# Splitting the second MLP weight matrix on GpSimd beside the attention, by way of a DRAM scratch

## The reference

```python
# attention: 2 batches x 8 heads, 768 rows, head size 64
mask = q_bucket[:, :, :, None] == k_bucket[:, :, None, :]   # buckets: signs of q @ proj and k @ proj, 6 bits
scores = np.where(mask, scale * (q @ k^T), -1e9)
attn = exp(scores - max) / (sum + 1e-9);  x = attn @ v      # as 1536 tokens x 512
# MLP: w_in 512 x 2048, w_out 2048 x 512
h = x @ w_in
g = (a0 + a1*h + a2*h^2 + a3*h^3) / (1 + |b0|*|h| + |b1|*h^2 + 1e-6)
x2 = g @ w_out
# experts: each token goes to the one of 8 experts with the highest logit
out = gate * sigmoid(x2 @ w_output_gate) * (relu(x2 @ w1[e]) @ w2[e])
```

## Time and profile before

| | us |
|---|---|
| median of three runs | 840.91 |
| lowest, highest | 838.65, 841.00 |
| the profiled execution | 839.78 |
| its span, first to last instruction | 837.9 |
| TensorE busy | 784.2 (94%) |
| VectorE busy | 661.4 (79%) |
| ScalarE busy | 586.8 (70%) |
| GpSimd busy | 346.9 (41%) |
| mean granted TensorE clock | 0.979 of full speed |

### The profile page before, as it was taken

The page is one execution under the profiler, slowest core; times in us unless marked ns, Lnnn a source line. Parts: engine busy times, 40 slices in busy tenths (PEclk is TensorE's granted clock), DMA queues, the critical chain, the costliest instruction groups (busy, mean ns, idle before and its releaser), DMA issues.

```text
span 837.9 us, 16486 instructions
## 1 busy us (share of the span) xinstructions
PE 784.2 (94%) x5008; PEld 676.1 (81%) x5008; DVE 661.4 (79%) x1097; ACT 586.8 (70%) x1042; POOL 346.9 (41%) x320
## 2 busy tenths in 40 slices
PE   3599999999998799999999999999799999999995
PEld 2488888888887688899999999978588888888884
DVE  2477777777776699887878778767799999999982
ACT  1366766667676588886776777752599888888873
POOL 4055564664654222221221222220266656566452
PEclk9799999999999999999999999998899999999998
DMA  3566787786954421010010000023783112515940
GB/s 95 108 143 141 160 180 142 170 181 141 188 120 113 114 87 40 1 38 1 0 38 0 0 13 25 0 100 140 257 295 125 50 38 85 194 53 190 363 142 0
DMA packets 75652, 89.49 MB, mean 107 GB/s; under 512 B 34468, under 2 KB 51620, under 8 KB 75621
## 3 DMA queue, kind: packets, MB, share of 16 engines
q1 hardware_dynamic: 72580, 80.97, 36.1%
q0 software_dynamic: 3040, 8.13, 3.0%
HBM read 108.82 MB, written 8.18 MB: 140 GB/s over the span
## 4 chain that ended last, share of the span: by engine, by line
PE 87%; DVE 4%; issue 2%; ACT 2%; DMA 2%; SPq 1%; POOL 1%; DVEq 0%; POOLq 0%; ACTq 0%
PE ps_s L585 15%; PE ps_t L753 12%; PE ps_s L730 12%; PE ps_t L603 10%; PE ps_o L515 8%; PE ps_t L501 7%; PE ps_o L603 5%; PE ps_s L486 4%; PE ps_s L488 4%; PE ps_s L739 2%; PE ps_p L471 2%; PE ps_p L464 1%; DVE mask_st L991 1%; PE ps_o L717 1%; PE ps_p L644 1%
## 5 line engine op out<-in xcount | busy, mean ns | idle before, releaser
L1436 POOL TENSOR_TENSOR g_lo<-num_b,g_hi 128x384 fp32r<-128x384 f32 x64 | 65.7, 1027 | 214.4 <-ACT g_hi L869 131.8
L996 DVE TENSOR_REDUCE row_max<-ps_s 128x1 f32<-128x768 f32 x96 | 91.0, 948 | 58.5 <-PE ps_s L488 58.5
L585 PE MATMUL ps_s<-xT,win_hi 128*128 (+1 forms) x512 | 132.7, 340 | 0.0
L1273 DVE TENSOR_TENSOR w_lo<-w_raw,w_hi 128x1024 fp32r<-128x1024 f32 x76 | 124.8, 1699 | 2.3 <-ACT w_hi L924 0.6
L795 ACT ACTIVATE probs<-ps_s,exp_bias,exp_scale 128x768 f32<-128x768 f32 x96 | 95.4, 994 | 14.8 <-DVE exp_bias L1008 14.8
L801 ACT ACTIVATE probsT<-ps_t 128x384 f32<-128x384 f32 x96 | 47.4, 493 | 69.2 <-PE ps_t L501 69.2
L585 PEld LDWEIGHTS ps_s<-xT,win_hi 128*128 128x128 f32 x512 | 92.4, 188 | 3.7 <-issue 0.3
L585 PE MATMUL ps_s<-xT,win_lo 128*128 (+1 forms) x256 | 86.1, 336 | 0.0
L501 PE MATMUL ps_t<-ident,probs 128*128 128x128 f32 x576 | 81.3, 278 | 0.8 <-DVE probsT L1022 0.8
L486 PE MATMUL ps_s<-k_mask,q_mask 76*128 76x384 f32 x192 | 75.4, 393 | 4.7 <-issue 4.7
L515 PE MATMUL ps_o<-probsT,v_raw 128*64 128x128 f32 x1152 | 76.3, 277 | 1.9 <-DVE probsT L1022 1.9
(11 more groups left out here) (203 smaller groups left out, 1949.4 us busy)
## 6 DMA issues: line engine op xcount, KB each, us to landing
w_raw<-in_moe_w_dram SPq DMA_DIRECT2D x152, 512.0 KB
xT<-x_st SPq DMA_DIRECT2D x32, 192.0 KB, 3.8
scale_row<-row_inverse_scratch SPq DMA_DIRECT2D x32, 191.8 KB, 3.7
win_raw<-in_moe_w_in_dram SPq DMA_DIRECT2D x16, 256.0 KB, 4.2
x_sb<-in_moe_w_out_dram SPq DMA_DIRECT2D x16, 256.0 KB, 3.1
qk_raw<-in_q_dram SPq DMA_DIRECT2D x16, 192.0 KB, 3.3
qk_raw<-in_k_dram SPq DMA_DIRECT2D x16, 192.0 KB, 3.9
k_mask<-qkT_hi SPq DMA_DIRECT2D x16, 192.0 KB, 3.9
```

Source lines behind the costliest of these rows:

```text
L585: mm = pe.matmul(h_bank[f % 4], a[w], xT[:, c, blocks, l, :], start=(c == 0 and n == 0), stop=(c == CD - 1 and n == 2))
L996: dve.tensor_reduce(row_max[:, c:c + 1], ps_s[c % 2][:, :, 0:HALF], AX.XY, ALU.max).then_inc(maxed, 1)
L1273: dve.tensor_tensor(w1_lo[par][:, c, :], w1_raw[:, c, :], w1_hi[par][:, c, :].bitcast(F32), ALU.subtract).then_inc(w1_lo_made, 1)
```

## The change

GpSimd now splits w_out during the attention, one block a head (`split_wout`), behind `split_win`. SyncE loads the raw block (`load_wout_raw`, 256 KB) and stores the split block of the head before (`store_wout`, 512 KB) to a DRAM scratch `wout_split_scratch`, both behind `load_win` and ahead of the loads of q and k. There is one raw buffer and one split buffer, so GpSimd waits for the raw block and for the previous store to land. Behind the attention each block comes back in one 512 KB transfer: blocks 0 and 1 once the last scores are made, 2 to 5 behind `place_x` of head 14, 6 to 15 once the last x is placed. This order follows from the memory: `k_cross` is allocated beside the other score operands, so that blocks 0 to 5 lie over buffers that die with the last scores. ScalarE's and VectorE's 16 instructions each are gone from group 0, and `mlp_down` waits for the block's transfer (`wout_in[f]`).

```diff
+    wout_dram = nc.dram_tensor("wout_split_scratch", (NF, P, 2, DM), F32).ap()
...
                 q_cross = [sb(f"q_cross{i}", [P, S], F32R) for i in range(2)]
+                k_cross = [sb(f"k_cross{i}", [P, S], F32R) for i in range(2)]
...
+                wout_raw = sb("wout_raw", [P, DM])
+                wout_st = sb("wout_st", [P, 2, DM], F32R)
...
-                wout_hi = sb("wout_hi", [P, NF, DM], F32R)
-                wout_lo = sb("wout_lo", [P, NF, DM], F32R)
+                wout = sb("wout", [P, NF, 2, DM], F32R)
...
+            def load_wout_raw(f):
+                sp.dma_start(wout_raw[:], wout_rows[f]).then_inc(wout_raw_in, 16)
+
+            def store_wout(f):
+                sp.dma_start(wout_dram[f], wout_st[:].bitcast(F32)).then_inc(wout_out, 16)
...
                 if more or par == 0:
                     load_win(m + 1, 1 - par)
+                if m0 > 0:
+                    hold(sp, wout_split, m)
+                    store_wout(m - 1)
+                load_wout_raw(m)
                 if more and more_qk:
                     hold(sp, qk_turned, 2 * m + 6)
...
             def load_wout(f):
-                sp.dma_start(x2_sb[f % GT][:], wout_rows[f]).then_inc(wout_in[f % GT], 16)
+                sp.wait_ge(wout_out, 16 * (f + 1))
+                sp.dma_start(wout[:, f, :, :].bitcast(F32), wout_dram[f]).then_inc(wout_in[f], 16)
...
-            for f in range(GT):
+            sp.wait_ge(scored, QT * HEADS)
+            for f in range(2):
                 load_wout(f)
             sp.wait_ge(inverted, HEADS)
             store_inverse(1)
+            sp.wait_ge(wout_split, NF)
+            store_wout(NF - 1)
             sp.wait_ge(inv_out, 16 * HEADS)
             sp.wait_ge(x_scaled, HEADS - 1)
             load_scale(1)
+            sp.wait_ge(x_lo_made, START + HEADS - 1)
+            place_x(PAIRS - 1, 0)
+            for f in range(2, 6):
+                load_wout(f)
+            sp.wait_ge(x_lo_made, START + HEADS)
+            place_x(PAIRS - 1, 1)
+            sp.wait_ge(attended, BLOCKS * HEADS)
             for par in range(2):
-                sp.wait_ge(x_lo_made, START + HEADS - 1 + par)
-                place_x(PAIRS - 1, par)
-            for f in range(GT, NF):
-                sp.wait_ge(wout_lo_made, f - GT + 1)
+                sp.wait_ge(x_out[par], 16 * START + 32 * PAIRS)
+            for f in range(6, NF):
                 load_wout(f)
...
-                pe.wait_ge(wout_lo_made, f + 1)
+                pe.wait_ge(wout_in[f], 16)
...
-            def hi_of_wout(f):
-
-                act.wait_ge(wout_in[f % GT], 16 * (f // GT + 1))
-                act.activation(wout_hi[:, f, :], x2_sb[f % GT][:], ACT.Copy).then_inc(wout_hi_made, 1)
...
-            def lo_of_wout(f):
-
-                dve.wait_ge(wout_hi_made, f + 1)
-                dve.tensor_tensor(wout_lo[:, f, :], x2_sb[f % GT][:], wout_hi[:, f, :].bitcast(F32),
-                                  ALU.subtract).then_inc(wout_lo_made, 1)
...
+            def split_wout(i, par):
+
+                n = 2 * i + par
+                pool.wait_ge(wout_raw_in, 16 * (n + 1))
+                if n > 0:
+                    pool.wait_ge(wout_out, 16 * n)
+                pool.tensor_scalar(wout_st[:, 0, :], wout_raw[:], 1.0, 0.0, ALU.mult, ALU.add).then_inc(wout_hi_made, 1)
+                pool.wait_ge(wout_hi_made, n + 1)
+                pool.tensor_tensor(wout_st[:, 1, :], wout_raw[:], wout_st[:, 0, :].bitcast(F32),
+                                   ALU.subtract).then_inc(wout_split, 1)
+
             def attention_head(i, par, more):
...
                     split_win(i, par)
                     scale_x(*done)
                     add_eps(i, par)
+                split_wout(i, par)
                 if 2 * i + par > 0:
                     lo_of_x(*done)
```

More of the change, by code:

```diff
@@ L97, in fused_kernel @@
                 row_inv = sb("row_inv", [P, STEPS])
-                k_cross = [sb(f"k_cross{i}", [P, S], F32R) for i in range(2)]
                 v_raw = [sb(f"v_raw{i}", [P, QT, D]) for i in range(2)]
@@ L211, in fused_kernel @@
             "pT_hi_half", "attended", "x_hi_made", "x_lo_made"))
-        wout_in = [sem(f"wout_in{i}") for i in range(GT)]
-        (wout_hi_made, wout_lo_made, gates_in, h_made, abs_h_made, num1, num2, num3, ln_made,
+        wout_in = [sem(f"wout_in{i}") for i in range(NF)]
+        wout_raw_in, wout_hi_made, wout_split, wout_out = map(sem, (
+            "wout_raw_in", "wout_hi_made", "wout_split", "wout_out"))
+        (gates_in, h_made, abs_h_made, num1, num2, num3, ln_made,
          r0_made, dr_made, nr_made, g_made, g_hi_made, g_lo_made, down_made, acc_made, x2_act, x2_dve, x2_turned,
          x2T_made, logit_ps, logit_made) = map(sem, (
-            "wout_hi_made", "wout_lo_made", "gates_in", "h_made", "abs_h_made", "num1", "num2",
+            "gates_in", "h_made", "abs_h_made", "num1", "num2",
             "num3", "ln_made", "r0_made", "dr_made", "nr_made", "g_made", "g_hi_made", "g_lo_made", "down_made", "acc_made",
@@ L600, in mlp_down @@
                     rows = slice(m * P, (m + 1) * P)
-                    for n, (a, b) in enumerate(((g_hi[f % 4], wout_hi), (g_hi[f % 4], wout_lo),
-                                                (g_lo[f % 2], wout_hi))):
-                        mm = pe.matmul(acc_bank[m][:], a[:, rows], b[:, f, :], start=(f == 0 and n == 0),
+                    for n, (a, l) in enumerate(((g_hi[f % 4], 0), (g_hi[f % 4], 1), (g_lo[f % 2], 0))):
+                        mm = pe.matmul(acc_bank[m][:], a[:, rows], wout[:, f, l, :], start=(f == 0 and n == 0),
                                        stop=(f == NF - 1 and n == 2))
@@ L615, in mlp_down_last @@
                         pe.wait_ge(g_lo_made, NF * g + f + 1)
-                        for n, (a, b) in enumerate(((g_hi[f % 4], wout_hi), (g_hi[f % 4], wout_lo),
-                                                    (g_lo[f % 2], wout_hi))):
-                            mm = pe.matmul(acc_bank[m][:], a[:, rows], b[:, f, :], start=False,
+                        for n, (a, l) in enumerate(((g_hi[f % 4], 0), (g_hi[f % 4], 1), (g_lo[f % 2], 0))):
+                            mm = pe.matmul(acc_bank[m][:], a[:, rows], wout[:, f, l, :], start=False,
                                            stop=(f == NF - 1 and n == 2))
@@ L894, in mlp_step @@
                 from_hidden(g, f)
-                if first:
-                    if f == 1:
-                        x_hi(PAIRS - 1, 1)
-                    if f == 4:
-                        for par in range(2):
-                            act.wait_ge(x_out[par], 16 * START + 32 * PAIRS)
-                    for b in range(NF * f // TAIL, NF * (f + 1) // TAIL):
-                        hi_of_wout(b)
+                if first and f == 1:
+                    x_hi(PAIRS - 1, 1)
                 if not first and f in (5, 7, 9):
@@ L1133, in mlp_step @@
                 from_hidden(g, f)
-                if first:
-                    for b in range(NF * f // TAIL, NF * (f + 1) // TAIL):
-                        lo_of_wout(b)
                 if not first and f in (4, 6, 8):
```

## The result

The change made the kernel slower, by 0.9%, where a gain of 7 us was forecast.

The account below looks back on a forecast made before the run. TensorE was taken as the bound (87% of the chain), with time to win in group 0: -9.0 there, +2.3 queue, +0.2 last head, sum -6.5, forecast 833.8 us, range 830.3 to 841.0.

Parts of the forecast that it names:

- -7.8: Group 0, first to last down product: TensorE runs at 4.19 us a step without gaps, saving 7.8 us.
- -1.2: Ahead of group 0's first down product: without VectorE's 1.42 us subtraction the division and TensorE start 1.2 us earlier.
- 0.4 us of idling or less before the first down product: Sign in group 0: TensorE would idle 0.4 us or less there, against 1.64 us before.
- GpSimd and the issues: Attention: GpSimd's pair of 0.62 and 1.30 us costs nothing, 3 us cover left; SyncE's issues, 0.85 us a head, just fit.
- rival E: GpSimd's new instructions hold up VectorE's small operations, 1.9 us in each of 16 heads, giving 862 us; chance 0.01.
- The engines' price: Attention: the DMA engines need 2.2 us a head for the added 768 KB, with 3.2 us free.
- SyncE falls behind by 0.45 us a head: Attention: queue loop 15.6 us against TensorE's 15.14, over ten heads 4.5 us, less 2.2 cover: +2.3 us.
- rival A: The SyncE and DMA queue loop becomes the bound, at its wait for the inverses' landing; chance 0.09 mild, 0.11 full.
- halfway: Rival A's case halfway to the upper bound: 1.5 us a head costs 12.8 us, giving 844; at the bound 849.
- cover: TensorE's lead on masks in the attention: about 3.8 us, 1.6 used at once, 2.2 left for falling behind.
- rival B: Last head's inverses held up behind block loads and the last store, delaying the first `g_hi`: 836.4 us; chance 0.14.
- Heads over 15.3 us from the start: Sign in the attention that would show the forecast wrong; it expected 15.14 us until late, then 15.6.

Follow-up runs that it names:

- e1: Changed kernel without the attention's w_out work, except block 0 split and stored once; all sixteen loads read block 0: 832.63 us.
- e2: Changed kernel with all issues, waits and splits, but from head 1 on only 8 KB per raw load and store; sixteen loads read block 0: 831.43 us.
- e5: Changed kernel without SyncE's wait for the inverses' landing; scale rows come from a row written once with head 0's inverses: 832.01 us.
- e8: Changed kernel with the w_in block and raw w_out loads issued during the wait for the inverses' landing, the store left behind the scale rows: 834.24 us.
- e3: Changed kernel with the w_out store and raw load issued behind the load of v, during the wait for the inverses' landing: 839.91 us.
- e6: Changed kernel with half of each transfer from head 1 on, 256 KB stored and 128 KB loaded a head; sixteen loads read block 0: 835.18 us.
- e4: Changed kernel with ScalarE issuing the w_out store and raw load from its own DMA queue, in the fourth step of each head: 838.71 us.

## Why the prediction was wrong

**Group 0: right in kind, one term too large.** -7.8 was forecast between the first and the last down product and -7.56 came, with no idling between them. The -1.2 ahead of the first came to 0.2 (e1, counted from the landmark). The product ahead of the division did start 0.9 us earlier, but the gain was lost behind it. The 1.42 us that the prediction charged to the subtraction were partly a hold-up beside GpSimd's `scale_x`, and with the subtraction gone this fell on the next operation, which took 1.57 us for 0.61. And without that, `x_hi` of the last head, at 282.38 to 282.91 in e1, would have held `g_hi` (283.39) back all but 0.5 us. The step had named two instructions that would be gone and had not asked what is late next. The forecast of 0.4 us of idling or less before the first down product failed by this too: 1.46 in e1, 2.51 in the changed kernel. So the MLP's half was worth some 7.8 us and not 9.0 (medians: 6.4 in e1, 7.6 in e2, 7.9 in e5).

**GpSimd and the issues: right.** 0.62 and 1.28 us for the pair, 2.98 us of cover left, no harm to VectorE in the attention (rival E did not come: e2 has the same instructions at 831.43). The prediction's ground against E was too narrow, though: the operation of 0.15 us has one column and reads one tensor. Where VectorE read two tensors from SBUF beside a GpSimd operation that did the same, at the start of group 0, it took 1.57 us for 0.61 (e1). The issues cost 1.2 us a head from the scale rows to q (2.13 at the least before, 3.3 now), a little over the 0.85 forecast; e2 shows that this alone just fits.

**The engines' price: right.** 2.1 us a head against 2.2.

**The loop: this step failed, by its size.** It is the term "SyncE falls behind by 0.45 us a head", +2.3 us in the sum, where +14.3 came. The prediction let the inverses' store come 0.6 us later and the cycle stand at 15.6, 0.45 over TensorE. Against e2, which has everything but the bytes, the landing came 1.08 later, and 0.53 were added where the prediction had nothing: the issues from q to the inverses took longer with a fuller queue. In the head shown q's issue took 0.73 us instead of 0.61. e2 stands at 15.30, where TensorE still leads at times; with these, and 0.07 less from the scale rows to q, it is 16.84. So the forecast cycle of 15.6 was short by 1.24 us a head: 0.30 in its base of 15.0, 0.53 in the issues and 0.48 in the landing, less the 0.07. (Counted from the kernel before, the part behind the inverses' store grew by only 0.70 us, near the 0.6; but there it had room to shrink, as e1's 1.91 shows.) The cycle is 1.70 a head over TensorE instead of 0.45; ten heads make 17.0, and TensorE is 14.3 late. The 2.7 between the two would be the cover (forecast: 2.2), but it is only what is left over; the same reckoning leaves 3.5 in e8, 3.6 in e3, 4.2 in e6 and 5.8 in e4, so it is rough. The mechanism and its place were named, as rival A, with 1.1 us a head as the point from which it decides; 1.70 lies between its "halfway" (844) and its bound (849). It was given 0.11 with the reason that the new pieces are large. That reason holds for the engines' time and not for the landing, through which the loop closes. And the price was worked out as an addition to a loop believed to have 0.15 us of slack: there every error of one step is multiplied by ten heads, so the chance should have been far greater.

**The last head (rival B): less than half its price.** From the last attention group to the first down product e8 takes 15.36 us and e5 15.32, the changed kernel 16.45. Its chain shows where it lies:

```profile
287.27 5.15 DMA row_inverse_scratch<-row_inv
292.43 0.49 SPq L324
292.97 3.70 DMA scale_row<-row_inverse_scratch
```

The 3 KB store landed after 5.15 us, issued 3.7 us behind the first of two loads of 512 KB (283.57); in e8, with the same loads in the same place, the step took 3.60:

```profile
276.12 3.60 DMA row_inverse_scratch<-row_inv
```

It was forecast as 0.2 us and cost about 1.1. Why the landing was 1.5 us longer here than in e8 stays open.

**What was named as a sign, and came.** "Heads over 15.3 us from the start" came (17.6 us for the first of the ten, 16.84 in the mean), and TensorE's first idling for masks was at 120.80, before the 150 that the prediction set. The DMA share was 0.84 and not 0.93, since the same work was spread over a longer head; here a share that stayed under 1 while TensorE waited spoke for a loop and not for a full resource, as e5 then showed.

What stays open is why the issues between q and the inverses take longer in a full queue. The rows show it (9.70 us in e2, 9.91 in e6, 10.23 in the changed kernel, 10.30 in e5), in step with the bytes, but no run takes it apart.

## What to carry to other kernels

An in-order DMA queue that waits for a transfer of its own closes a loop: the time of its issues plus that landing is a pace of its own, and in these runs bytes added to the queue lengthened both the landing and the issues around it (e2, e6 and the changed kernel), at a mean share of the DMA engines under 0.85. Before putting work on such a queue, add up one cycle of it from the rows (issue to issue of the same line), compare with the bound engine's, and treat a slack of some tenths of a microsecond as none. If bytes must go there, issue during the landing wait those whose landing nobody needs soon, and keep the large ones behind the transfer that the next engine waits for; and look first for what can be won by order alone, which here was 3 us for two moved loads.

## What the runs showed that was not expected

- A 3 KB store to DRAM landed after 1.5 us (median) in e1, 1.6 in e2, 2.4 before and in e6, 2.7 in e3, 3.0 in the changed kernel, 3.3 in e8, 3.5 in e5 and 3.9 in e4. The mean share of the DMA engines from 120 to 240 us does not order them: 0.78 before, 0.79 in e2, 0.97 in e3, 0.98 in e5 and 0.87 in e4. What is in flight at its moment seems to count for more; e4, with ScalarE's issues beside the store, fits that.
- VectorE's `inv_b` and `num_b` operations of 128x384 with two inputs in SBUF took 0.56 to 0.62 us, and 1.46 to 1.57 us where they fell beside GpSimd's `scale_x` (e1, e2, e5, e8).
- A second queue gave the small store no way past large transfers issued at the same moment: its landing was longest there, 3.9 us (e4).
- With a share of 0.97 over 100 to 240 us, and of 1.02 within it, the attention ran as fast in e5 as with 0.78 before. Full DMA engines did not by themselves bound it.
